# Sparse attention ahead of two expert layers on one core: the global scores of all eight heads in one block, earlier in each batch

## The reference

```python
# q_l, k_l, v_l: 4 batches x 8 heads x 512 positions x 64; q_g, k_g, v_g: 32 positions
k_all = concat([k_g, k_l]); v_all = concat([v_g, v_l])
out_g = softmax(scale * q_g @ k_all.T) @ v_all        # global queries see all 544 keys
s_ll  = where(|i - j| <= 32, scale * q_l @ k_l.T, -1e9)  # local queries: a window
s_lg  = scale * q_l @ k_g.T                               # and the 32 global keys
out_l = softmax(concat([s_lg, s_ll])) @ v_all
x = concat([out_g, out_l]) laid out as 2304 tokens x 512
# then a soft mixture of 8 experts (logits, two softmaxes, w1, relu, w2),
# and last h = x @ w_in; g = h - tanh(h); g @ w_out
```

## Time and profile before

| | |
|---|---|
| median of 3 runs | 319.38 us (318.92 to 320.33) |
| profiled execution | 318.87 us, of it span 317.1 us |
| granted TensorE clock, mean | 0.999 |
| busy: PE, DVE, ACT, POOL | 306.9, 211.9, 139.0, 64.8 us |
| attention loop begins | 14.59 us |
| attention, last weighing over | 111.79 us |

### The profile page before, as it was taken

The page is one execution under the profiler, slowest core; times in us unless marked ns, Lnnn a source line. Parts: engine busy times, 40 slices in busy tenths (PEclk is TensorE's granted clock), DMA queues, the critical chain, the costliest instruction groups (busy, mean ns, idle before and its releaser), DMA issues.

```text
span 317.1 us, 7840 instructions
## 1 busy us (share of the span) xinstructions
PE 306.9 (97%) x2987; PEld 220.3 (69%) x2987; DVE 211.9 (67%) x443; ACT 139.0 (44%) x293; POOL 64.8 (20%) x62
## 2 busy tenths in 40 slices
PE   7999999999999999999998999999999999999994
PEld 4576777777777786233335888788888888888883
DVE  3887988888889556721258877566556666566572
ACT  1366766666566642111137554432334222532531
POOL 0543434434335001000008964000000000000000
PEclk9999999999999999999999999999999999999999
DMA  7999999999999969999999000030003000300202
GB/s 236 376 375 341 334 377 407 370 401 372 375 390 343 391 232 378 414 407 412 415 419 406 21 2 0 1 132 2 0 0 134 0 0 0 135 1 0 99 2 74
DMA packets 18032, 69.56 MB, mean 219 GB/s; under 512 B 4176, under 2 KB 5840, under 8 KB 14288
## 3 DMA queue, kind: packets, MB, share of 16 engines
q1 hardware_dynamic: 18000, 69.14, 57.7%
HBM read 64.41 MB, written 4.46 MB: 217 GB/s over the span
## 4 chain that ended last, share of the span: by engine, by line
PE 86%; DVE 7%; issue 5%; ACT 1%; POOL 1%; DVEq 0%; POOLq 0%
PE ps L846 20%; PE ps L849 20%; PE ps L550 6%; PE ps L595 5%; PE ps L821 5%; PE ps L746 4%; PE ps L777 4%; PE ps L587 3%; PE ps L566 3%; DVE sc L1101 3%; PE ps L606 2%; PE ps L541 2%; PE ps L560 2%; PE ps L581 2%; PE ps L658 1%
## 5 line engine op out<-in xcount | busy, mean ns | idle before, releaser
L849 PE MATMUL ps<-wlo,gg 128*128 128x512 f32 x204 | 80.5, 395 | 0.0
L846 PE MATMUL ps<-whi,gg 128*128 128x512 f32 x204 | 80.3, 394 | 0.0
L1307 DVE SCALAR_TENSOR_TENSOR nt<-uu,ps 128x512 f32<-128x512 f32 (+2 forms) x80 | 48.4, 607 | 47.3 <-ACT uu L1008 47.1
L1008 ACT ACTIVATE uu<-ps 128x512 f32<-128x512 f32 (+2 forms) x80 | 42.8, 537 | 84.0 <-PE ps L821 78.2
L457 POOL TENSOR_TENSOR sc<-sc,mx 128x640 f32<-128x640 f32 x32 | 40.1, 1253 | 53.5 <-DVE mx L1106 53.5
L1318 DVE TENSOR_TENSOR gg<-nt,ps 128x512 fp32r<-128x512 f32 (+2 forms) x80 | 47.9, 601 | 0.1
L846 PEld LDWEIGHTS ps<-whi,gg 128*128 128x128 f32 x204 | 38.4, 188 | 8.8
L849 PEld LDWEIGHTS ps<-wlo,gg 128*128 128x128 f32 x204 | 38.4, 188 | 8.0
L1101 DVE TENSOR_TENSOR sc<-ps,cst 128x640 f32<-128x640 f32 x32 | 26.2, 820 | 7.5 <-PE ps L550 5.9
L821 PE MATMUL ps<-cT,Pst 128*128 128x512 f32 (+2 forms) x80 | 28.9, 361 | 0.7 <-DVE Pst L1289 0.6
L595 PEld LDWEIGHTS ps<-vv,eT 128*64 128x64 f32 x512 | 18.7, 137 | 13.4 <-issue 11.0
(11 more groups left out here) (130 smaller groups left out, 384.6 us busy)
## 6 DMA issues: line engine op xcount, KB each, us to landing
w<-moe_w SPq DMA_DIRECT2D x11, 2048.0 KB, 11.2
vv<-v_t SPq DMA_DIRECT2D x8, 1170.0 KB, 7.7
w<-moe_w SPq DMA_DIRECT2D x14, 512.0 KB, 11.6
kT<-k_t SPq DMA_DIRECT2D x16, 416.0 KB, 6.3
out<-oo SPq DMA_DIRECT2D x17, 256.0 KB, 2.2
qT<-q_t SPq DMA_DIRECT2D x16, 256.0 KB, 7.3
win<-moe_w_in SPq DMA_DIRECT2D x4, 1024.0 KB, 16.6
wout<-moe_w_out SPq DMA_DIRECT2D x3, 1024.0 KB, 22.2
```

The costliest lines, as they stand in the source:

```text
L846: pe.matmul(o, g, hi, start=(c == 0), stop=False)
L849: mm = pe.matmul(o, g, lo, start=False, stop=(c == NC - 1))
L1008: nc.scalar.activation(uu[c % 2][:, 0:width], cols(h_bank(i, c), width), ACT.Square, scale=(1.0 / 3) ** 0.5).then_inc(square_ready, 1)
L1307: nc.vector.scalar_tensor_tensor(out=nt[c % 2][:, 0:width], in0=uu[c % 2][:, 0:width], scalar=1.0, in1=cols(h_bank(i, c), width), op0=ALU. ...
```

## The change

All global scores of a batch are now computed in one block at k=0 of the same batch: eight matmuls of 512 columns (two units alternating), then eight of 32. The output rows of the second unit are placed so that all eight use different pieces (64 rows x 32 columns) of the array: `global_rows`. Unit 4 uses banks 0 and 1, unit 9 banks 2 and 3. Each has its own buffer `scg` and `gmx`. VectorE takes both out ahead of normalising unit 0. The other blocks move: k=1 units 5, 6; k=3 units 7, 8; k=5 and k=7 as before the next batch's 0, 1 and 2, 3. Nothing global stands ahead of the loop. The DMA order follows.

```diff
+        def rank(k):
+            return k if k < 5 else 5 if k == 9 else k + 1
+        def global_rows(qd, j):
+            return 32 * (j ^ qd)
...
         AHEAD = 5
-        SCORES_AT = {(u - AHEAD) % U: u for u in (0, 2, 4, 5, 7, 9)}
+        SCORES_AT = {5: 0, 7: 2, 0: 4, 1: 5, 3: 7}
...
-                sp.wait_ge(scores_ready, U * (i - 1) + GQ[pr // 2] + 1)
+                sp.wait_ge(scores_ready, U * (i - 1) + (6, 6, 8, 10)[pr])
...
                 queries(i + 1, 1)
+                global_queries(i + 1)
+                keys(i + 1, 2)
+                queries(i + 1, 2)
                 load_w1(sp, i - 1, w1_loaded, w1s[i - 1][:])
-                keys(i + 1, 2)
                 keys(i + 1, 3)
-                global_queries(i + 1)
+                queries(i + 1, 3)
                 values(i + 1, 0)
-                queries(i + 1, 2)
-                queries(i + 1, 3)
...
+                pe.wait_ge(masked_ready, U * i + rank(k))
...
+                    for j in range(4):
+                        for qd in range(2):
+                            one(qd, j, 0)
+                    for qd in range(2):
                         for j in range(4):
...
+                            mm = one(qd, j, 1)
+                        mm.then_inc(scores_ready, 1)
...
             turn_probs(1, 0)
-            wake_for_scores(1, 4, cst)
-            scores(4)
             with pe.Fori(1, NB) as i:
...
+                    if k == 0:
+                        global_maxima(i)
                     normalise(i, k)
-                    if k + 5 < U:
-                        maxima(i, k + 5)
-                    elif not last:
+                    if 1 <= k <= 4:
+                        maxima(i, k + 4)
+                    elif 5 <= k <= 8 and not last:
                         maxima(i + 1, k + 5 - U)
```

More of the change, by code:

```diff
@@ L297, in probs_of @@
         def probs_of(k):
-            return scg if k in GQ else pr[k % 2]
+            return scg[k // 5] if k in GQ else pr[k % 2]
         def lowered(i, k):
@@ L354, in _ @@
             keys(1, 2)
+            keys(1, 3)
             queries(1, 2)
-            keys(1, 3)
             queries(1, 3)
@@ L530, in scores, with one @@
             def scores(k):
-                bank = scores_ps(k)
                 if k in GQ:
-                    for part in range(2):
-                        for j in range(4):
[L536 to L542, removed]
+                    def one(qd, j, part):
+                        pr = 2 * qd + j // 2
+                        r = slice(64 * (j % 2), 64 * (j % 2) + 64)
+                        own = kT[pr][r, 0:768].rearrange("r (b n) -> r b n", n=96)[:, :, 0:64]
+                        keys = kT[pr][r, 768:768 + SG] if part else own
+                        at = global_rows(qd, j)
+                        o = ps[at:at + 32, scores_ps(GQ[qd]) + part, 0:SG if part else 512]
+                        return pe.matmul(o, qgT[r, pr, :], keys, start=True, stop=True)
+                    for j in range(4):
+                        for qd in range(2):
+                            one(qd, j, 0)
+                    for qd in range(2):
+                        for j in range(4):
+                            mm = one(qd, j, 1)
+                        mm.then_inc(scores_ready, 1)
                 else:
@@ L612, in batch @@
                     u = SCORES_AT.get(k)
-                    if last and u is not None and u < AHEAD:
+                    if last and k >= AHEAD:
                         u = None
@@ L1084, in _, with global_maxima @@
             dve.wait_ge(mask_loaded, 16)
-            def maxima(i, k):
-                dve.wait_ge(scores_ready, U * i + k + 1)
-                h = head_of(k)[2]
-                if k in GQ:
-                    dve.wait_ge(probsT_ready, U * i + k - 4)
+            def global_maxima(i):
+                for qd in range(2):
+                    k = GQ[qd]
+                    dve.wait_ge(scores_ready, U * i + rank(k) + 1)
+                    dve.wait_ge(probsT_ready, U * (i - 1) + k + 1)
                     dve.sem_inc(passed_by_dve, 1)
@@ new lines, in global_maxima, with maxima @@
+                        scg[qd][:], cols(scores_ps(k), SL + SG), cst[:, C_ZERO:C_ZERO + 1].broadcast_to([P, SL + SG]),
+                        1.0, -3.0e38, ALU.add, ALU.max, gmx[qd][:, 0:1]).then_inc(masked_ready, 1)
+                for qd in range(2):
+                    dve.wait_ge(masked_ready, U * i + rank(GQ[qd]) + 1)
+                    nc.vector.tensor_scalar(gmx[qd][:, 1:2], gmx[qd][:, 0:1], -SCALE, None, ALU.mult).then_inc(gmax_ready, 1)
+            def maxima(i, k):
+                dve.wait_ge(scores_ready, U * i + rank(k) + 1)
+                h = head_of(k)[2]
+                dve.wait_ge(exp_ready, U * i + (unit_of(h - 2) if h >= 2 else unit_of(h + 6) - U) + 1)
+                bank = scores_ps(k)
+                nc.vector.tensor_tensor(sc[h % 2][:].rearrange("p (b n) -> p b n", b=2),
+                                        ps[:, bank:bank + 2, 0:320],
+                                        cst[:, C_MASK:C_MASK + 640].rearrange("p (b n) -> p b n", b=2),
+                                        ALU.add).then_inc(masked_ready, 1)
+                dve.wait_ge(masked_ready, U * i + rank(k) + 1)
+                nc.vector.tensor_reduce(mx[h % 2][:], sc[h % 2][:].rearrange("p (j n) -> p j n", j=4),
+                                        AX.X, ALU.max).then_inc(max_ready, 1)
```

55 lines of the change are left out of this document (20 added, 35 removed).

## The result

The changed kernel takes 321.98 us (median of 13 runs, 321.05 to 324.16) against 319.14 us for the kernel before in the same comparison (13 runs, 318.30 to 320.83). The ratio is 1.0092, 95% interval 1.0074 to 1.0110: slower, by 2.8 us. The forecast was 322.7 us, in a range of 320.3 to 326.6.

A forecast was written before the change was run, and what follows sets the result against it. Attention was taken to be held by TensorE's work with VectorE hard behind. Start -0.5, inner batches +1.2 and last batch +2.6 gave +3.3 us: 318.87 became 322.2, stated as 322.7 for the median, range 320.3 to 326.6.

The forecast's parts named there:

- the prediction's own signs of being wrong: Turning of unit 6 finds its copies done, or a load is what TensorE waits for.
- Part 1: TensorE's global block: eight matmuls in flight take 1.15 us instead of 2.10 for two blocks; batch work 23.92 to 22.97.
- Rival A: Global block: only four of eight matmuls work at a time, 2.10 us, +3.8 us, 326.5 us; chance 0.13.
- The rule of the Trainium skill: Different row tiles cannot access one PSUM bank at once, so the block would take turns; the sum of a 326.5 us case.
- Part 2: Ahead of the loop: block and waking matmul go, unit 1 turned at 14.08 instead of 14.59; -0.5 us.
- Part 5: DMA queue: later key requests cost nothing; if the cover failed, a microsecond or two in the first batch.
- Part 3: Inner batches: later scores of units 5 to 8 add waits, 2.51 us a batch; +0.4 three times, +1.2 us.
- The walk's times: Inner batch from k=0: mask of unit 5 at 6.58, scores 7 and 8 at 10.23, turning unit 6 at 14.08.
- Part 4: Last batch: score blocks +0.1, waits 3.4 against about 0.4 before, 0.5 off for no register work; +2.6 us.
- Rival B: Attention: saved TensorE work counts, latency is covered, waits stay 1.0 us a batch; -3.3 us, 316.1 us; chance 0.09.
- rival C: Attention: waits half of those walked, 1.8 us a batch and 1.7 in the last; +0.5 us, 319.9 us; chance 0.07.

The follow-up runs named there:

- run 1: Changed kernel with the block's two global units one after the other, four matmuls in flight: 323.66 us, ratio 1.0144 to the kernel before.
- run 5: Changed kernel with w1's load issued behind the next batch's first values and spread_global(i,0): 322.32 us, ratio 1.0104 to the kernel before.
- run 12: Changed kernel; in the last batch alone VectorE takes out units 5 to 8 ahead of normalising units 1 to 4: 322.59 us, ratio 1.0089 to the kernel before.
- run 3: Changed kernel with two 512-column filler matmuls on TensorE behind weighing unit 5 in the last batch: 323.12 us, ratio 1.0116 to the kernel before.
- run 6: Changed kernel with the block moved behind unit 9 of the batch before, loads ordered as in the kernel before: 323.06 us, ratio 1.0112 to the kernel before.
- run 2: Changed kernel with w1's load moved to the front of a batch's loads: 327.84 us, ratio 1.0257 to the kernel before.
- run 4: Changed kernel with VectorE taking out unit 6 ahead of normalising unit 2 in every batch: 323.31 us, ratio 1.0125 to the kernel before.
- run 9: Changed kernel with unit 6 taken out ahead of normalising unit 2 and w1's load behind first values and spread_global(i,0): 323.24 us, ratio 1.0114 to the kernel before.
- run 10: Kernel before with VectorE taking out scores behind units 1 and 6 ahead of normalising them, and w1's load behind the first values: 321.80 us, ratio 1.0079.
- run 7: Changed kernel, block behind unit 9, old load order, VectorE taking out scores behind units 1 and 6 before normalising them: 317.95 us, ratio 0.9973 to the kernel before.
- run 8: Kernel before with only VectorE taking out scores behind units 1 and 6 ahead of normalising those units: 317.97 us, ratio 0.9954.

## Why the prediction was right, and where its steps were off

The verdict and the size came out, and so did the mechanism in the last batch, where the loss is. One of the prediction's own signs of being wrong came out too: a load is among what TensorE waits for. Step by step:

- **Part 1, the block: right.** 1.08 us for 1.15; eight in flight, and 1.98 when made to go in series (run 1). Rival A is out. The rule of the Trainium skill (TensorEngine Tiling, Restrictions and Gotchas, Gotcha 1) doesn't describe this kernel: with both row halves writing each bank, at different partitions, the block takes 1.08 us, little more than half of the serial one.
- **Part 2, ahead of the loop: the -0.5 did not come.** In the changed kernel's profile unit 1 was turned at 14.58, since the very first score block took 2.07 us instead of 1.32, which no change of the code explains (see the last section). In run 5, with 1.32, it is turned at 13.94, as walked (14.08), but then TensorE waits 0.38 us for keys, and the first block starts at 16.34, as in the changed kernel (16.33). All four key loads must be there by then: Part 5's "a microsecond or two in the first batch" was the right place.
- **Part 3, the inner batches: right in kind, too dear.** Predicted +0.4 each, measured -0.1, +0.15 and, without the load wait, +0.1. The walk's times, from turning unit 1 (moved by the 0.36 of the load in batch 3): mask of unit 5 at 6.58, measured 71.69 - 65.17 = 6.52; scores of units 7 and 8 at 10.23, measured 10.09, but only 0.36 of it waited (0.65 walked), no more than before; turning unit 6 at 14.08, measured 13.61. The step off is mostly the last link. I took 1.87 us from exponential to the end of the copies, from the earlier trace rows, where ScalarE had to wait for TensorE's transposes between them; when ScalarE is what is late, they are ready, and it takes 1.47 (77.16 to 78.63).
- **Part 4, the last batch: right, the largest term.** Predicted +2.6; measured +2.3 in run 5 and +2.5 in run 12 (91.67 to 114.95) from first to last weighing, and +3.0 in the changed kernel with the 0.74 that no chain explains. Its waits are written as 3.4 where the terms named sum to 3.3. The cause is the one given, too little TensorE work beside the chain; runs 3, 6 and 12 show it from three sides.
- **Part 5, the loads at nothing: wrong.** The value loads cost 1.1 us in the profiled execution. How much of it is in the median stays open: the spread of the executions (3.1 us) is larger, and run 5, without these waits, has no lower median. What the runs do show is that loads were a second bound right behind the first (runs 2, 4, 9, 10).
- **Rival B fell** although TensorE has 2.7 us less to do, **rival C** (319.9) lies below every execution.

Two of the steps failed in opposite directions (Part 3 by 1.1 us too much, Parts 2 and 5 by up to 1.6 too little), so the closeness of 322.7 to 321.98 is partly luck. Of the 2.8 us between the medians, 2.3 to 2.5 are the last batch and about 0.1 the three before it, by the profiles; for the rest, some 0.3, loads are the likely cause, but no run shows it.

**Both kernels are beaten** by runs 7 and 8: 1.1 us below the kernel before, 4.0 below the changed one, by the medians. The edit that pays is VectorE's order. The merged block adds nothing to it in the end. In the two profiles it saves 1.2 us in the first batch (24.01 against 25.21), 0.2 and 0.4 in the next two (24.05 against 24.26 and 24.47) and 1.6 in the last, mostly the value wait that run 8's has; its start costs 3.6 (unit 1 turned at 17.50 against 13.93). About 1.2 us of that are the first score blocks, which came late in run 7's execution (the second starts at 11.42 against 10.23), so the profiles don't settle what the block is worth without it.

## What to carry to other kernels

Work taken from the busiest engine is a gain only where no chain of the others ends there. Compare, from each produced tile to its use, the chain's length with the busy engine's work in between: here 7.1 us of chain met 7.7 us of work before and 5.0 after, and it was the straight-line last batch, without work for a next one, that paid. Then look at the loads: with a DMA share of 1.0 every microsecond won in a batch is asked of the queue as well, and one 2 MB load, moved either way in the queue, cost between nothing and 5.9 us in four runs (runs 2, 5, 9 and 10, each against the kernel without the move) and gained in none.

## What the hardware showed that I had not expected

- TensorE runs eight 64x32 pieces at once with pairs of row halves on one bank: 1.08 us for what takes 1.98 in series.
- After TensorE had stood for 1.8 us (run 6) the granted clock was 0.79 on average from 16 to 24 us, after 2.3 us (run 10) 0.71 from 56 to 64 us, and single pieces took 1.3 to 2.0 times as long. In run 7's profiled execution the same stand of 1.8 us left it at 1.00 over the same 8 us. What decides between them stays open. Run 7's window:

```profile
16.00:24.00 8.00, 7.84 (x130) 1.00 1.00 341
```

- The executions of one program can fall into two groups with 1.3 us between their medians (run 8). A wait for values of 1.4 us, seen in one of the upper group, is of that size; no execution of the lower group was profiled.
- The very first score block took 1.32 us in five of the 14 profiled executions and 1.47 to 2.25 in the others, of the same code; the kernel before had the short one in its profile, the changed kernel one of 2.07. The traces' records of the granted clock begin, at full speed, at 5.1 to 6.1 us in the five and at 6.5 to 8.1 in the others, and a block starting at 6.12 is the longer the later that is. That fits a block which ran at the half clock until then (a whole one at half speed takes 2.41, run 10); what ran ahead of the first record the views don't show.
